# Routed experts on one core: tile 0's outputs last, the other tiles' outputs inside the branch, the next row count loaded before them

## The reference, cut to what matters

```python
attn_out = _attn_ref(r, k, v, w, u)              # recurrence over 768 steps, 2 x 8 heads of 48
x = attn_out.transpose(0, 2, 1, 3).reshape(1536, 384)
x = relu(x @ w_in) ** 2 @ w_out                  # 384 -> 2048 -> 384
logits = x @ w_gate                              # 8 experts
e = argmax(logits, axis=1); p = softmax(logits)[n, e]
# each expert takes its tokens in order, at most capacity = 384 of them
out[n] = p * (relu(x[n] @ w1[e]) @ w2[e])        # 384 -> 1024 -> 384, 0 for tokens over the cap
```

## Time and profile before

| | us |
|---|---|
| median of 3 runs | 458.02 (458.01 to 459.62) |
| the profiled execution | 458.81, its span 457.1 |
| TensorE busy | 431.2 |
| VectorE busy | 309.7 |
| ScalarE busy | 255.3 |
| GpSimd busy | 57.8 |
| share of TensorE in the chain that ended last | 82% |

### The profile page before, as it was taken

One profiled execution on the slowest core, in us unless ns is written; L12 is line 12 of the kernel. 1 busy time (PEld: TensorE's weight loads), 2 busy tenths in 40 slices (PEclk: granted clock), 3 DMA queues, 4 the chain that ended last, 5 costly groups with the idle time before them and its releaser, 6 DMA issues.

```text
span 457.1 us, 14532 instructions
## 1 busy us (share of the span) xinstructions
PE 431.2 (94%) x5882; PEld 409.5 (90%) x5882; DVE 309.7 (68%) x763; ACT 255.3 (56%) x527; POOL 57.8 (13%) x78
## 2 busy tenths in 40 slices
PE   2789999999999999999999999999999999999994
PEld 2678899999999999999999999998997789999994
DVE  4787966757686769677867737558556877678510
ACT  2164866456645654565545566575448876686421
POOL 7300000000000100001000200221020333321201
PEclk9999999999999999999999999999999999999998
DMA  8717795880130015001000157431966998610001
GB/s 275 274 60 238 261 325 183 284 329 4 49 145 4 2 44 185 3 1 39 3 1 3 40 209 275 142 120 27 315 215 208 313 353 275 206 61 0 32 1 44
DMA packets 35642, 63.39 MB, mean 139 GB/s; under 512 B 3980, under 2 KB 21950, under 8 KB 35568
## 3 DMA queue, kind: packets, MB, share of 16 engines
q1 hardware_dynamic: 33264, 57.88, 37.3%
q0 software_dynamic: 2304, 4.47, 2.6%
HBM read 50.77 MB, written 14.19 MB: 142 GB/s over the span
## 4 chain that ended last, share of the span: by engine, by line
PE 82%; DVE 6%; issue 5%; ACT 2%; DMA 2%; POOL 1%; POOLq 0%; SPq 0%; DVEq 0%; ACTq 0%
PE bank L718 21%; PE bank L704 19%; PE pair L625 6%; PE bank L931 6%; PE bank L884 5%; PE pair L586 3%; PE pair L884 3%; PE pair L899 3%; PE bank L938 3%; PE bank L899 3%; DVE AD L1224 2%; PE pair L644 2%; DVE KS L1215 2%; DMA stage<-in_moe_w_in 2%; PE pair L679 1%
## 5 line engine op out<-in xcount | busy, mean ns | idle before, releaser
L704 PE MATMUL bank<-XH,W 128*128 128x256 f32 x576 | 118.6, 283 | 0.9 <-ACT RB L1073 0.9
L718 PE MATMUL bank<-W,GH 128*128 128x384 f32 x372 | 98.4, 345 | 0.0
L704 PEld LDWEIGHTS bank<-XH,W 128*128 128x128 f32 x576 | 94.9, 189 | 1.9 <-issue 1.2
L704 PE MATMUL bank<-XL,W 128*128 128x256 f32 x288 | 80.6, 280 | 0.0
L718 PEld LDWEIGHTS bank<-W,GH 128*128 128x128 f32 x372 | 61.7, 188 | 1.3
L1073 ACT ACTIVATE RB<-bank 128x256 f32<-128x256 f32 x96 | 36.7, 382 | 46.6 <-PE bank L704 45.9
L718 PE MATMUL bank<-W,GL 128*128 128x384 f32 x186 | 62.6, 337 | 0.0
L1276 DVE TENSOR_TENSOR GL<-GG,GH 128x256 fp32r<-128x256 f32 x96 | 40.6, 423 | 32.0 <-ACT GH L970 31.5
L970 ACT ACTIVATE GH<-GG 128x256 fp32r<-128x256 f32 x96 | 40.1, 418 | 35.9 <-PE bank L718 34.4
L1215 DVE TENSOR_TENSOR KS<-KS 128x512 f32<-128x512 f32 x72 | 50.3, 699 | 8.8 <-PE pair L625 8.8
L704 PEld LDWEIGHTS bank<-XL,W 128*128 128x128 f32 x288 | 54.3, 188 | 0.0
(11 more groups left out here) (165 smaller groups left out, 716.5 us busy)
## 6 DMA issues: line engine op xcount, KB each, us to landing
raw<-in_moe_w SPq DMA_DIRECT2D x23, 768.0 KB, 7.5
stage<-in_moe_w SPq DMA_DIRECT2D x9, 768.0 KB, 8.1
KS<-in_krw SPq DMA_DIRECT2D x12, 512.0 KB, 5.9
slots<-X SPq DMA_DIRECT2D x8, 579.0 KB, 6.6
VV<-in_v SPq DMA_DIRECT2D x12, 288.0 KB, 6.9
KS<-in_krw SPq DMA_DIRECT2D x12, 256.0 KB, 6.1
stage<-in_moe_w_in SPq DMA_DIRECT2D x4, 768.0 KB, 7.0
stage<-in_moe_w_out SPq DMA_DIRECT2D x4, 768.0 KB, 7.2
```

The lines of the kernel that those rows point to most:

```text
L704: last = nc.tensor.matmul(bank[4 + f % 2][:, 0:2 * P], win[wa][:, c, f * P:(f + 1) * P], xa[:, c, :], start=n == 0, stop=n == 3 * KM - 1)
L718: last = nc.tensor.matmul(bank[6 + m][:, 0:DM], ga[(NF * g + f) % G3][:, cols], wout[wa][:, f, :], start=f == 0 and n == 0, stop=f == NF - ...
```

## The change: what it does

On TensorE the short branch now also has `rows_in(e + 1, 1)` and `rows_in(e + 1, 2)` and the increments for tiles 1 and 2 (through `hidden_small` with m = 0). In the long branch `outputs2(e, 2)` follows `hidden_small(e, 2, ...)`, and `outputs2(e, 1)` follows for both ways of it, with `rows_in(e + 1, 2)` between its halves. Behind the branches come the load of the next expert's count and `outputs2(e, 0)`, which waits once for four steps of HH or HL instead of once for each. ScalarE's weighted outputs and GpSimd's scatters take the order 2, 1, 0.

```diff
             for e in range(NE):
-                for m in range(MT):
+                for m in reversed(range(MT)):
                     pool.wait_ge(yo_ready[m], e + 1)
...
                     last.then_inc(done, NFE // 2)
+                rows_in(e + 1, 1)
+                if m == 0:
+                    rows_in(e + 1, 2)
 
             def outputs2(e, m):
...
+                high, low = (hh3_ready, hl3_ready) if m == MT - 1 else (hh_ready, hl_ready)
                 for c in range(2):
                     fs = range(c * NFE // 2, (c + 1) * NFE // 2)
-                    if m == 0:
-                        pe.wait_ge(wl_ready, NW0 + CH * e + CH // 2 + c + 1)
-                        if c == 1:
-                            pe.wait_ge(hl_ready, NFE * (e + 1))
-                            rows_in(e + 1, 2)
+                    pe.wait_ge(wl_ready, NW0 + CH * e + CH // 2 + c + 1)
+                    if m == 1 and c == 1:
+                        pe.wait_ge(hl_ready, NFE * (e + 1))
+                        rows_in(e + 1, 2)
                     for f in fs:
-                        if m == 0:
-                            pe.wait_ge(hh_ready, NFE * e + f + 1)
-                        elif m == MT - 1:
-                            pe.wait_ge(hh3_ready, NFE * e + f + 1)
+                        if m > 0:
+                            pe.wait_ge(high, NFE * e + f + 1)
+                        elif f == fs[0]:
+                            pe.wait_ge(high, NFE * e + fs[-1] + 1)
...
+            def rows_of_expert(e):
+                return pe.value_load(count_u[0:1, e:e + 1]) if e < NE else None
+
+            rows = rows_of_expert(0)
             for e in range(NE):
-                rows = pe.value_load(count_u[0:1, e:e + 1])
                 with pe.If(rows <= P):
                     hidden_small(e, 0, h2_done)
                     pe.sem_inc(h3_done, NFE)
+                    pe.sem_inc(y2_done[2], 1)
+                    pe.sem_inc(y2_done[1], 1)
                 with pe.Else():
                     hidden2(e)
                     with pe.If(rows > 2 * P):
                         hidden_small(e, 2, h3_done)
+                        outputs2(e, 2)
                     with pe.Else():
                         rows_in(e + 1, 0)
                         pe.sem_inc(hs_done, 2)
                         pe.sem_inc(h3_done, NFE)
-                rows_in(e + 1, 1)
+                        pe.sem_inc(y2_done[2], 1)
+                        rows_in(e + 1, 1)
+                    outputs2(e, 1)
+                rows = rows_of_expert(e + 1)
                 outputs2(e, 0)
-                with pe.If(rows > P):
-                    outputs2(e, 1)
-                    with pe.If(rows > 2 * P):
-                        outputs2(e, 2)
-                    with pe.Else():
-                        pe.sem_inc(y2_done[2], 1)
-                with pe.Else():
-                    pe.sem_inc(y2_done[1], 1)
-                    pe.sem_inc(y2_done[2], 1)
...
-                weighted(e, 0)
                 with act.If(rows > P):
-                    weighted(e, 1)
                     with act.If(rows > 2 * P):
                         weighted(e, 2)
                     with act.Else():
                         act.sem_inc(yo_ready[2], 1)
+                    weighted(e, 1)
                 with act.Else():
+                    act.sem_inc(yo_ready[2], 1)
                     act.sem_inc(yo_ready[1], 1)
-                    act.sem_inc(yo_ready[2], 1)
+                weighted(e, 0)
```

More of the change, by code:

```diff
@@ L933, in outputs2 @@
                     for f in fs:
[L934 to L937, removed]
+                        if m > 0:
+                            pe.wait_ge(low, NFE * e + f + 1)
+                        elif f == fs[0]:
+                            pe.wait_ge(low, NFE * e + fs[-1] + 1)
                         last = nc.tensor.matmul(y, HL[:, f, cols], w2s(e, 0)[:, f, :], start=False, stop=f == NFE - 1)
                 last.then_inc(y2_done[m], 1)
+            def rows_of_expert(e):
+                return pe.value_load(count_u[0:1, e:e + 1]) if e < NE else None
+            rows = rows_of_expert(0)
             for e in range(NE):
-                rows = pe.value_load(count_u[0:1, e:e + 1])
                 with pe.If(rows <= P):
```

## The result

The kernel after takes 474.71 us (median of 4 runs, 473.09 to 477.01), the kernel before beside it 458.01 (4 runs, 457.0 to 459.62). The ratio is 1.0351, 95% interval 1.0318 to 1.0383: slower. The prediction was 471.3, from 461.5 to 477.5. The profiled execution took 474.92 us with a span of 473.1, which is 16.0 more than the span before.

The account below looks back on a forecast made before the run. TensorE, busy 94%, was taken to bound the kernel, standing still at branches into instruction pages not yet fetched. Stalls +9.3, clock +3.9 and the rest +0.1 gave +13.3 us on 458.0: 471.3 us, range 461.5 to 477.5.

Parts of the forecast that it names:

- The place of the wait: Jump ending the short branch, over 343 instructions: long page wait in experts 1, 2 and 3, cheap in expert 5.
- S: Stall at each long jump of experts 1 to 3: 3.4 to 5.7 us, middle 4.55; 3S - 4.3 = +9.3 us.
- The clock: TensorE's clock falls in the rests of experts 1 to 3, costing 1.3 us each, +3.9 us for three.
- the first term: Few-row experts on TensorE: three stalls S less the waits of today that go away, +9.3 us.
- the 0.1 for the rest: Many-row experts, scatters and the end of the kernel together: +0.1 us.
- The cover: Only short transposes are queued ahead of the new jump, next to no cover; today's outputs cover 3.1 us.
- What was costed at nothing: Tile 2's outputs right behind its transposes, waiting for HH and HL: 0 in expert 0, +0.05 us in expert 7.
- The far jump served in time: Rival 1: more pages held or count off, S 0.3 at the long jumps, -4.9 us, 453.1; chance 0.12.
- A clock that holds: Rival 3: pages as forecast, but TensorE's clock does not fall in the rests, 467.4 us; chance 0.20.
- The one of the page asked for at the branch: Rival 2: missed page requested at the branch, 2.7 to 3.8 us, no clock fall, +5.4, 463.4 us; chance 0.17.
- my own reading: Entering a page of 256 instructions fetches the next and no other; a jump into it waits until it has landed.
- The gain of the change: Waits of today around experts 1 to 3 that go away: 4.3 us in the sum.

Follow-up runs that it names:

- The two padded kernels: The kernel after with never-executed padding making each expert 512 instructions, and two amounts of padding ahead: one page boundary per jump 458.89 us, two boundaries 479.18 us.
- the light loads: The kernel after with the later experts' weight loads cut to 32 columns of each chunk, TensorE's instructions the same: 470.88 us.
- the hinted kernel: The kernel after with a prefetch hint at the head of the short branch for the jump at its end: 457.81 us, ratio 0.9988.
- the useless hint: The kernel before with a prefetch hint ahead of tile 0's outputs for the branch of L956 behind them: 458.85 us, ratio 0.9995.
- the kernel before, aligned: The kernel before with 59 never-executed increments in the part L956 jumps over and 16 more before the experts: 463.01 us, ratio 1.0088.
- the first padded one: The kernel after with 38 never-executed increments in each long branch and 16 more before the experts, one page boundary per jump: 458.89 us, ratio 1.0009.
- the kernel with cover: The kernel after with tile 0's outputs copied into both branches, ahead of the jump, and 64 more increments before the experts: 463.75 us, ratio 1.0092.

## Why the prediction was right

**The place of the wait: right.** All four jumps stood where the count put them, three dear, one cheap (0.293). A packet of q8 moved in each long one. The two padded kernels differ in where the boundaries stand (and in 96 increments ahead of the experts, which move the first load of a count by 0.7 us) and in 20.3 us of time, which settles that it is they.

**S, 4.55 forecast, 4.87 measured (5.15, 4.82, 4.64): mis-sized by 0.96 us in all.** I had bounded it by 3.4 with the queues idle and 5.7 with them full and taken the middle, since the queues should be less full. The lower bound holds: 3.26 in an idle stretch. During the jumps the DMA share was 0.60 to 0.69, so nearer to full than I took it for. The term is +10.3 for +9.3.

**The clock, 1.3 forecast for a rest, 1.9 measured: mis-sized, +5.7 for +3.9.** That it falls in such a rest was right. I took a third of the 4.2 us of outputs because no row of before had matmuls at 1.2 GHz. Measured, some 4 us of the work behind the rest ran at half speed, so about 2 us were lost: near one half, not a third. With the first term's 1.0 these 1.8 us make up the 2.7 by which the forecast sum of 13.3 fell short of 16.0; the 0.1 for the rest is not to be seen. That three falls cost the same 1.9 us is not a rule: the light loads had 1.4 to 2.8.

**The cover: right.** TensorE had 10 short transposes ahead and stopped for 5.11 us of 5.15. The kernel with the outputs ahead of the jump shows what cover is worth: about 2.5 us a jump, where the forecast counted on 3.1, and no fall of the clock in two of three.

**What was costed at nothing: right.** In expert 0 and expert 7 the outputs of tile 2 follow the transposes without a wait for HH or HL, as in these rows of the timeline, which answer to the earlier trace rows and to the last ones of the earlier trace rows:

```profile
328.78 1.64 PE L934 MATMUL pair<-W,HH 128*128 128x384 f32 x8
330.26 0.86 PE L941 MATMUL pair<-W,HL 128*128 128x384 f32 x4
...
453.93 0.66 PE L911 MATMUL pair<-ident,under_HL 128*128 128x128 f32 x4 [0.25 <-ACT under_HL L973]
454.52 1.63 PE L934 MATMUL pair<-W,HH 128*128 128x384 f32 x8
```

**The rivals.** The far jump served in time is out: 4.6 to 5.1 us, and its -4.9 us was too good even so (next paragraph). A clock that holds is out by the windows. The one of the page asked for at the branch was half right: in the unhinted kernel the packet moves 2.2 to 2.7 us after the jump begins, and the hinted kernel shows that nobody asks sooner. Its price of 2.7 to 3.8 us was not, because in the kernel before those branches were waiting for a page already asked for. There my own reading, from the entry to the page, is what the useless hint bears out. The Trainium skill, "Runtime: NRT & Kernel Launch", section "Instruction fetch mechanics", has the blocks of 256 instructions that these runs show; its room for 2048 instructions did not keep a jump of 343 from missing.

**The gain of the change: half of what the sum has.** It did remove the rests between the experts, 3.5 us (1.13, 1.71 and 0.68), for which the sum has 4.3 with the loads behind them. But the new order costs something by itself, which no term of mine has. Where no page is waited for, a short expert, from its first matmul to that of the next, takes 10.51 and 10.73 us in the old order (experts 1 and 2 of the kernel before, aligned) and 10.86 to 10.98 in the new (experts 1 to 3 of the hinted kernel, 1 and 2 of the first padded one): TensorE now rests 0.30 to 0.43 us before the outputs, for HH. From the first load of a count to the last matmul the profiled runs take 138.5 us before and 136.3 hinted. So the change, freed of its stalls, wins 2.2 us in the stage, in one run each. The time doesn't show it (457.81 against 458.26): the profiled run of the hinted kernel lost 1.3 us ahead of the experts, for a reason that stays open, and the runs vary by more than what is left (456.36 to 459.53 in eight of its ten, 461.71 and 464.48 in the others).

## What to carry to other kernels

In a long program without loops, number the instructions and mark the page ends before moving code between branches: a jump that skips a whole page waits 3.3 to 5.1 us for its target (once 6.4), where a shorter one, with the next page in time, takes 0.3 to 0.4. Leave queued work ahead of such a jump (4.2 us of outputs hid about 2.5 of each here), or ask for its target early, from within the same page; and compare two orders of work only with their page alignment in view, since alignment alone moved this kernel by 20 us. Check straight code too: with weight loads filling the DMA queues, the page that comes next in order can be late.

## What the runs showed of the hardware that I had not expected

- Straight code waits for its page: 5.32 us between two transposes, with DMA over 100% busy and the page's packet behind it. All eleven traces have such a stop at 22 to 24 us, 2.53 us in the kernel after.
- TensorE goes on 2.3 to 2.8 us after the page's packet starts to move, in 32 branches of 32; full queues lengthen only the time before the packet, from 0.9 to 3.9 us.
- A page nobody has asked for costs 3.26 us (13% DMA share), 3.50 to 3.77 (16 to 20%), 4.6 to 5.1 (60 to 72%) and once 6.37 (101%). The share over the whole jump is a rough guide: in the kernel with cover the first jump took 3.61 at 60%, its packet moving 0.9 us in.
- TensorE's granted clock stayed at 1.00 over rests of 1.95 and 1.45 us, and fell to 0.50 in or behind every rest of 3.2 us and more; in the kernel after it stayed there for 6.8 us each time, of which 4 had matmuls.
- A prefetch hint takes 31 to 50 ns and hid the whole fetch where the jump was in its page, six of six times; with a page end between the two it did nothing, in two of two layouts, and for the next page in order it won nothing.
